# A routed expert layer: zero rows during the last MLP block, unused slots between used ones, and the halves of neighbouring slots interleaved

## The reference

```python
def phi(x):                                   # linear attention, 4 x 8 heads, 576 x 64
    proj = np.einsum('bhsd,df->bhsf', x, w_phi)
    proj = proj - np.max(np.abs(proj), axis=-1, keepdims=True)
    return np.concatenate([np.exp(proj), np.exp(-proj)], axis=-1)
q_p, k_p = phi(q), phi(k)
kv = np.einsum('bhsf,bhsd->bhfd', k_p, v); z = np.sum(k_p, axis=2)
x = (q_p @ kv) / (q_p @ z + 1e-6)             # -> 2304 tokens x 512
h = x @ w_in                                  # dense MLP, 512 -> 2048 -> 512
y = (h * np.clip(h + 3.0, 0.0, 6.0) / 6.0) @ w_out
e_idx = np.argmax(y @ w_gate, axis=1)         # 8 experts, top 1
for e in range(8):                            # 512 -> 1024 -> 512
    m = e_idx == e
    out[m] = gate[m, None] * eom[m, e, None] * (np.maximum(y[m] @ w1[e], 0) @ w2[e])
```

## Time and profile before

| | us |
|---|---|
| runs | 967.49, 962.7, 963.38; median 963.38 |
| profiled execution | 964.04 |
| its span (first to last instruction) | 962.5 |
| PE busy | 869.5 (90%) |
| DVE busy | 580.6 (60%) |
| ACT busy | 388.8 (40%) |
| POOL busy | 74.9 (8%) |

### The profile page before, as it was taken

How to read it: one execution, slowest core, us unless ns; L and a number is a source line. 1 busy time by engine, 2 the same in 40 slices (tenths; PEclk the granted TensorE clock), 3 DMA queues, 4 the chain that set the end, 5 groups by cost and what they waited for, 6 DMA issues and landing times.

```text
span 962.5 us, 20311 instructions
## 1 busy us (share of the span) xinstructions
PE 869.5 (90%) x7480; PEld 574.2 (60%) x7481; DVE 580.6 (60%) x1202; ACT 388.8 (40%) x666; POOL 74.9 (8%) x120
## 2 busy tenths in 40 slices
PE   5999999998899999997999999992499999999990
PEld 3777777777455555553555555552377777777770
DVE  3778788875795987985987987545131322222223
ACT  2445456656456565664656665522010100011011
POOL 1000000000000001001001001011011111111111
PEclk9999999999999999998999999995599999999995
DMA  6243344331565366465266452554317342664110
GB/s 191 92 161 113 132 160 161 128 123 36 192 235 202 143 234 223 162 230 216 97 226 224 156 206 121 201 182 150 103 46 299 137 162 98 228 251 176 44 34 13
DMA packets 44062, 151.36 MB, mean 157 GB/s; under 512 B 7710, under 2 KB 12062, under 8 KB 37856
## 3 DMA queue, kind: packets, MB, share of 16 engines
q1 hardware_dynamic: 38320, 134.14, 39.2%
q0 software_dynamic: 5520, 16.31, 4.9%
q10 hardware_dynamic: 160, 0.07, 0.0%
HBM read 104.72 MB, written 47.21 MB: 158 GB/s over the span
## 4 chain that ended last, share of the span: by engine, by line
PE 57%; PEld 14%; DVE 10%; issue 8%; DMA 4%; PEldq 3%; ACT 2%; SPq 1%; DVEq 0%; POOL 0%; POOLq 0%; ACTq 0%
PE ps L743 19%; PE ps L732 17%; PEld ps L834 10%; PE ps L607 4%; PE ps L634 4%; PE ps L673 3%; PEld ps L846 3%; DVE arena L1087 3%; PE ps L834 2%; PE ps L648 2%; DVE arena L1094 2%; PE ps L846 2%; DMA arena<-split 1%; DVE u_mx L1253 1%; PE ps L661 1%
## 5 line engine op out<-in xcount | busy, mean ns | idle before, releaser
L732 PE MATMUL ps<-arena,w_in_sb 128*128 128x384 f16 x1152 | 203.5, 329 | 6.0 <-issue 6.0
L743 PE MATMUL ps<-w_out_sb,arena 128*128 128x512 f16 x576 | 172.3, 381 | 9.1 <-DVE stage L1341 9.1
L732 PEld LDWEIGHTS ps<-arena,w_in_sb 128*128 128x128 f16 x1152 | 111.4, 99 | 81.7 <-issue 9.2
L1067 ACT ACTIVATE w_in_sb<-ps 128x512 f16<-128x512 f32 x50 | 29.5, 597 | 257.0 <-PE ps L834 241.3
L834 PEld LDWEIGHTS ps<-w_in_sb,arena 128*128 128x128 f16 x2112 | 124.0, 100 | 9.8 <-issue 5.0
L834 PE MATMUL ps<-w_in_sb,arena 128*128 128x128 f16 x2112 | 125.9, 223 | 4.3 <-DMA arena<-split 2.4
L846 PE MATMUL ps<-arena,w_in_sb 128*128 128x512 f16 x528 | 117.5, 379 | 0.0
L743 PE MATMUL ps<-w_out_sb,stage 128*128 128x512 f16 x288 | 109.7, 381 | 0.0
L1442 DVE SCALAR_TENSOR_TENSOR w_in_sb<-ps,w_in_sb 128x512 f16<-128x512 f32 x50 | 34.3, 691 | 113.7 <-ACT w_in_sb L1067 113.7
L743 PEld LDWEIGHTS ps<-w_out_sb,arena 128*128 128x128 f16 x576 | 55.9, 98 | 68.9 <-issue 11.7
L1033 ACT ACTIVATE arena<-relu 128x384 f16<-128x384 f32 x96 | 50.2, 523 | 106.6 <-DVE relu L1336 106.6
(11 more groups left out here) (175 smaller groups left out, 927.5 us busy)
## 6 DMA issues: line engine op xcount, KB each, us to landing
arena<-in_moe_w SPq DMA_DIRECT2D x16, 2048.0 KB, 13.1
split<-arena SPq DMA_DIRECT2D x16, 2048.0 KB, 7.4
arena<-split SPq DMA_DIRECT2D x32, 1024.0 KB, 5.8
arena<-in_qkt SPq DMA_DIRECT2D x15, 576.0 KB, 6.2
stage<-in_moe_w_in SPq DMA_DIRECT2D x16, 512.0 KB, 4.3
stage<-in_moe_w_out SPq DMA_DIRECT2D x16, 512.0 KB, 5.4
w_in_sb<-rows POOLq DMA_DIRECT2D x25, 257.0 KB, 3.0
arena<-in_v SPq DMA_DIRECT2D x32, 128.0 KB, 4.5
```

The costliest lines, as they stand in the source:

```text
L732: last = nc.tensor.matmul(ps[:, HB[f % GB], 0:BN], w_in_sb[:, lw, c, f * P:(f + 1) * P], xt[:, a, c, lx, :], start=c == 0 and lw + lx == 0 ...
L743: last = nc.tensor.matmul(ps[:, YB + r, :], g_sb[lg_][:, f % GB, r * P:(r + 1) * P], w_out_sb[:, lw, f, :], start=f == 0 and lg_ + lw == 0 ...
```

## The change

1. The zero rows of an expert are written as soon as the positions of the last block but one are known: `padrow` is taken in the last MLP block, SP writes 512 rows (`BN + P`) behind each expert's row count so far, and POOL makes the last scatter only when they have landed. `REGION` grows by `BN`. POOL makes `zrow` before its last but one scatter.
2. The tables put the unused slots at positions 2, 4, 6 and so on, as many as there are; `slot_at` is the number of a position among the used ones. The tables that are read later (`slot_inv`) are made behind the release.
3. PE's slot is cut in `hidden_step` and `output_step`. The order is hidden(s + 1), transposes(s + 2), output(s). The output step reads the three table values again. DVE's and POOL's orders follow.
4. w1 of an expert is loaded when the last hidden step of expert e - 2 is done, w2 as before by `eo_done`.

```diff
-REGION = N + P
+REGION = N + BN + P
...
                 load_expert(1, 0, half)
+            sp.wait_ge(zrow_ready, 1)
+            sp.wait_ge(pad_ready, 1)
+            for e in range(E):
+                row = sp.value_load(padrow[0:1, e:e + 1], min_val=0, max_val=DUMMY - BN - P)
+                sp.dma_start(rows[bass.ds(row, BN + P), :].rearrange("(p r) w -> p r w", p=P),
+                             zrow[:, None, :].to_broadcast([P, BT + 1, XW // 2])).then_inc(zeroed, 16)
             sp.wait_ge(y_step, BLOCKS * FC)
             for half in range(2):
                 load_expert(1, 1, half)
 
-            sp.wait_ge(dummy_stored, 16)
-            sp.wait_ge(pad_ready, 1)
-            for e in range(E):
-                row = sp.value_load(padrow[0:1, e:e + 1], min_val=0, max_val=DUMMY - P)
-                sp.dma_start(rows[bass.ds(row, P), :], zrow[:]).then_inc(zeroed, 16)
             sp.wait_ge(table_ready, 1)
             for e in range(2, E):
                 free = sp.value_load(free_at[0:1, e:e + 1], min_val=1, max_val=SLOTS + 1)
+                free1 = sp.value_load(free_w1[0:1, e:e + 1], min_val=1, max_val=2 * SLOTS + 1)
+                sp.wait_ge(eh_done, free1)
+                for half in range(2):
+                    load_expert(e, 0, half)
                 sp.wait_ge(eo_done, free)
                 for half in range(2):
-                    for m in range(2):
-                        load_expert(e, m, half)
+                    load_expert(e, 1, half)
...
-            step(nc.gpsimd.iota(iota_s[:], [[1, SLOTS], [0, E]], base=0, channel_multiplier=0, allow_small_or_imprecise_dtypes=True))
+            step(nc.gpsimd.iota(iota_s[:], [[1, SLOTS]], base=0, channel_multiplier=0, allow_small_or_imprecise_dtypes=True))
+            step(nc.gpsimd.iota(half_s[:], [[1, (SLOTS + 1) // 2], [0, 2]], base=0, channel_multiplier=0, allow_small_or_imprecise_dtypes=True))
+            step(nc.gpsimd.memset(gap_s[:], float(SLOTS + 1)))
+            step(nc.gpsimd.iota(gap_s[:, 2:SLOTS:2], [[1, SLOTS // 2]], base=1, channel_multiplier=0, allow_small_or_imprecise_dtypes=True))
...
-            scatter(BLOCKS - 2)
             pool.wait_ge(x_transposed, BLOCKS * DC)
             step(nc.gpsimd.memset(zrow[:, 0:DM + 1], 0.0))
-            step(nc.gpsimd.iota(zrow[:, DM + 1:DM + 2].bitcast(I32), [[0, 1]], base=NOWHERE, channel_multiplier=1))
-
+            nc.gpsimd.iota(zrow[:, DM + 1:DM + 2].bitcast(I32), [[0, 1]], base=NOWHERE, channel_multiplier=1).then_inc(zrow_ready, 1)
+            pool.wait_ge(zrow_ready, 1)
             pool.dma_start(rows[DUMMY:DUMMY + P, :], zrow[:]).then_inc(dummy_stored, 16)
+            scatter(BLOCKS - 2)
+            pool.wait_ge(zeroed, 16 * E)
             scatter(BLOCKS - 1)
             pool.wait_ge(table_ready, 1)
-            pool.wait_ge(zeroed, 16 * E)
             pool.wait_ge(dummy_stored, 16)
             pool.wait_ge(scattered, 16 * TILES)
...
+            next_load(0, 0)
             with pool.Fori(0, (SLOTS - 3) // 2) as i:
                 for a in range(2):
-                    next_load(i * 2 + a, a)
+                    next_load(i * 2 + (a + 1), 1 - a)
                     store(i * 2 + a, a)
-            next_load(SLOTS - 3, 0)
...
+            pe.drain().then_inc(eh_done, 1)
...
-            def slot(s, a, turn, more=True):
+            def hidden_step(s, a, turn, more=True):
...
                 if more:
                     slot_transposes(s + 1, 1 - a, turn + a)
+
+            def output_step(s, a):
+                parity = pe.value_load(slot_par[0:1, bass.ds(s, 1)], min_val=0, max_val=1)
+                used = pe.value_load(slot_used[0:1, bass.ds(s, 1)], min_val=0, max_val=1)
+                need = pe.value_load(slot_need[0:1, bass.ds(s, 1)], min_val=32, max_val=32 * E)
                 pe.wait_ge(ew2_loaded, need)
                 if not isinstance(s, int) or s > 1:
                     pe.wait_ge(og_ready, s - 1)
...
-            slot(0, 0, 1)
-            slot(1, 1, 1)
-            with pe.Fori(0, (SLOTS - 3) // 2) as i:
-                slot(i * 2 + 2, 0, i + 2)
-                slot(i * 2 + 3, 1, i + 2)
-            slot(SLOTS - 1, 0, SLOTS // 2 + 1, False)
+            hidden_step(0, 0, 1)
+            hidden_step(1, 1, 1)
+            output_step(0, 0)
+            hidden_step(2, 0, 2)
+            output_step(1, 1)
+            with pe.Fori(1, (SLOTS - 3) // 2) as i:
+                hidden_step(i * 2 + 1, 1, i + 1)
+                output_step(i * 2, 0)
+                hidden_step(i * 2 + 2, 0, i + 2)
+                output_step(i * 2 + 1, 1)
+            hidden_step(SLOTS - 2, 1, SLOTS // 2)
+            output_step(SLOTS - 3, 0)
+            hidden_step(SLOTS - 1, 0, SLOTS // 2 + 1, False)
+            output_step(SLOTS - 2, 1)
+            output_step(SLOTS - 1, 0)
 
 
         @block.scalar
...
                 for j in range(2):
-                    act.wait_ge(eh_done, s * 2 + (j + 1))
+                    act.wait_ge(eh_done, s * 2 + (j + 2))
...
+                            nc.vector.tensor_copy(padrow[:], base[:, 0, :]).then_inc(pad_ready, 1)
                     if f not in (0, FC - 1):
                         gate_lo(n, f)
...
+            link(nc.vector.tensor_scalar(unused[:], cnt[:, src, E - 1:E], -1.0, float(SLOTS), ALU.mult, ALU.add))
+            nc.vector.tensor_scalar(slot_gap[:], gap_s[:], unused[:, 0:1], float(2 * SLOTS), ALU.is_le, ALU.mult)
+            link(nc.vector.scalar_tensor_tensor(out=slot_at[:], in0=half_s[:, 0:SLOTS], scalar=unused[:, 0:1], in1=iota_s[:],
+                                                op0=ALU.min, op1=ALU.subtract))
+            link(nc.vector.tensor_tensor(slot_at[:], slot_gap[:], slot_at[:], ALU.subtract))
+
+            link(nc.vector.tensor_tensor(sl[:, 0], slot_at[:, :, None].to_broadcast([P, SLOTS, E]), upto, ALU.is_ge))
             link(nc.vector.tensor_tensor(sl[:, 1], sl[:, 0], upto, ALU.mult))
...
+            link(nc.vector.tensor_scalar(unused_before[:, 2:E], cnt[:, src, 0:E - 2], -2.0, 0.0, ALU.add, ALU.max))
...
+            link(nc.vector.scalar_tensor_tensor(out=unused_before[:, 2:E], in0=unused_before[:, 2:E], scalar=unused[:, 0:1],
+                                                in1=cnt[:, src, 0:E - 2], op0=ALU.min, op1=ALU.add))
+            nc.vector.tensor_scalar(slot_need[:], slot_count[:], 32.0, 32.0, ALU.mult, ALU.add)
+            nc.vector.tensor_scalar(free_w1[:, 2:E], unused_before[:, 2:E], 2.0, 1.0, ALU.mult, ALU.add)
+            link(nc.vector.tensor_scalar(free_at[:, 2:E], unused_before[:, 2:E], 1.0, None, ALU.add))
+            nc.vector.tensor_tensor(e_inv[:], u_pow[:].rearrange("p (e m) -> p e m", m=2)[:, :, 0],
+                                    u_pow[:].rearrange("p (e m) -> p e m", m=2)[:, :, 1], ALU.mult).then_inc(table_ready, 1)
...
             slot_in(0, 0)
-            slot(0, 0, None)
-            slot(1, 1, None)
-            with dve.Fori(0, (SLOTS - 3) // 2) as i:
-                slot(i * 2 + 2, 0, i + 1)
-                slot(i * 2 + 3, 1, i + 1)
-            slot(SLOTS - 1, 0, SLOTS // 2, False)
+            slot_lo(0, 0)
+            slot_in(1, 1)
+            slot_lo(1, 1)
+            slot_in(2, 0)
+            slot_out(0, 0, None)
+            slot_lo(2, 0)
+            slot_in(3, 1)
+            slot_out(1, 1, None)
+            with dve.Fori(1, (SLOTS - 3) // 2) as i:
+                slot_lo(i * 2 + 1, 1)
+                slot_in(i * 2 + 2, 0)
+                slot_out(i * 2, 0, i)
+                slot_lo(i * 2 + 2, 0)
+                slot_in(i * 2 + 3, 1)
+                slot_out(i * 2 + 1, 1, i)
...
```

More of the change, by code:

```diff
@@ L145, in moe_program @@
         slot_par, slot_used, slot_need, parity_i, slot_row, slot_token = (table(SLOTS).bitcast(I32) for _ in range(6))
+        slot_at, slot_gap, slot_count = (table(SLOTS) for _ in range(3))
         og_token = table(2).bitcast(I32)
@@ L175, in moe_program @@
         free_at = sb("free_at", [P, E], I32)
+        free_w1 = sb("free_w1", [P, E], I32)
+        unused = sb("unused", [P, 1])
+        unused_before = sb("unused_before", [P, E])
         expert8 = sb("expert8", [P, E])
@@ L187, in moe_program @@
         cnti = sb("cnti", [P, E], I32)
-        iota_s = sb("iota_s", [P, SLOTS, E])
+        iota_s = sb("iota_s", [P, SLOTS])
+        half_s = sb("half_s", [P, SLOTS + 1])
+        gap_s = sb("gap_s", [P, SLOTS])
         carrier = sb("carrier", [1, 2])
@@ L265, in moe_program @@
         scattered = sem("scattered")
+        zrow_ready = sem("zrow_ready")
         zeroed = sem("zeroed")
@@ L1410, in _ @@
-            link(nc.vector.scalar_tensor_tensor(out=slr[:, 2, :], in0=slr[:, 0, :], scalar=float(REGION), in1=slr[:, 1, :], op0=ALU.mult, op1=ALU.add))
-            link(nc.vector.tensor_scalar(slot_used[:], slr[:, 0, :], float(E), None, ALU.is_lt))
-            link(nc.vector.tensor_scalar(slr[:, 0, :], slr[:, 0, :], float(E - 1), None, ALU.min))
```

(42 more changed lines are left out.)

23 lines of the change are left out of this document (7 added, 16 removed).

## The result

The changed kernel takes 1020.17 us, median of 4 runs (1018.18 to 1020.67), against 963.04 for the kernel before beside it (4 runs, 960.31 to 967.49): ratio 1.0585, 95% interval 1.0542 to 1.0628. The forecast was 1002 with a range of 978 to 1020: right in sign, 18 us short, and at the very edge of its range (0.2 us above its upper end, where the runs themselves spread over 2.5 us). The profiled execution has a span of 1019.0 us, 56.5 more than before.

The account below looks back on a forecast made before the run. PE was taken as busy throughout each used slot (10.99 us) at full clock, with three losses around the slots. The terms summed to +38.9 us on the 962.5 us span, 1001.4, forecast as 1002 us, range 978 to 1020.

Parts of the forecast that it names:

- Term 1: Before 18 outputs that directly follow hidden and transposes: three uncovered value loads idle PE 1.7 us each, +30.6 us.
- R2: Rival: loads ahead of the output are covered, wholly (970 us) or half (986 us); chance 0.12 for both.
- Term 2: Before the hidden step of slot 1, now directly after its transposes: its three loads cost +1.7 us once.
- Terms 3 and 4: Unused positions 2, 4, 6: uncovered loads and drains, +20.8 us; slower clock after four long idle stretches there, +7.8 us.
- Term 5: Late weights of expert 2: w1 is asked for earlier, so the whole loss goes, -4.0 us.
- Term 6: End of the kernel: with a used output last, 24.5 us after its evacuation become 9.8, -14.7 us.
- Term 7: Transition from MLP to slots: earlier but four times larger zero DMAs bring the first row load 3.3 us sooner.
- R4: Rival: zero rows bound the transition at 250 GB/s, +6 instead of -3.3, 1011 us; chance inside the forecast's 0.65.
- R1: Rival: the clock also falls in the regular gaps before outputs, 1017 us, or 1032 if all; chance 0.15.
- R3: Rival: faster, with output loads covered and unused positions skipped cheaply while other work is queued, 945 us; chance 0.05.

Follow-up runs that it names:

- run 1: The kernel before, with PE reading the three table values a second time between transposes and output matmuls: 993.01 us, ratio 1.0355.
- run 2: The changed kernel with the three values packed in one word and both steps' words read ahead of the hidden matmuls: 977.32 us, ratio 1.0183 to the kernel before.
- run 7: As run 2, with one-column matmuls in place of `drain` as an unused slot's signal: 978.56 us, ratio 1.0144 to the kernel before.
- run 8: Run 7 with 128 zero rows late, issued from two queues, and unused slots at 8, 10 and 12: 964.48 us, ratio 1.0009 to the kernel before.
- run 12: Run 8 with an unused slot's hidden step no longer waiting for DVE's copy of its rows: 958.72 us, ratio 0.9950 to the kernel before.
- run 3: The changed kernel with the unused slots put last again: 1013.85 us, ratio 1.0563 to the kernel before.
- run 5: The kernel before with only the changed order of weight loads, w1 first: 958.49 us, ratio 0.9950.
- run 4: The kernel before with the early zero rows alone, 512 per expert: 969.79 us, ratio 1.0116.
- run 6: The changed kernel with the early zero rows undone, 128 per expert written when the last positions are known: 1016.06 us, ratio 1.0546 to the kernel before.
- run 9: The kernel before with w1 first and the eight zero DMAs issued from two queues, SP and ACT: 956.14 us, ratio 0.9921.
- run 11: Run 8 with the unused slots last instead of at 8, 10 and 12: 964.99 us, ratio 1.0024 to the kernel before.

## Why the prediction was right, and where it was short

The step that makes the change slow was forecast as it came: three loads without cover ahead of each regular O. The misses of the other terms nearly all point the same way, so no error hides another; they add up to the 18 us that put the result at the edge of the range.

**Term 1, loads ahead of O (+1.7 a slot).** Right in mechanism and size: +1.79 in the change, +1.70 with the loads alone (run 1), nothing with the loads moved (run 2). This is the larger half of the loss. Every regular gap, 1.41 to 1.86 us, lies in the bracket of 1.2 to 2.1; none has half the price, so R2 falls, whole and half. The Trainium skill (TensorE: Matmul & The Clock Gate, the table of specifications) gives TensorE's queue a depth of 64; no cover beyond the 17 pairs read from the earlier trace rows shows in these gaps.

**Term 2, H(1).** 2.29 for 1.7, and another mechanism: not its loads but DVE's copy of slot 1, which I had put "beside it". The three loads are done at 704.1, the copy ends at 704.88, and the branch is taken at 705.0 (the same in run 2). That the size was near is luck.

**Terms 3 and 4, unused positions and clock.** Forecast 20.8 and 7.8, together 28.6; measured 23.8 of idle (3.24 + 8.17 + 1.74 + 4.38 + 1.90 + 4.38) and 9.3 of slower matmuls, 33.1. Position by position the double one at 765 (6.3 and 2.3 behind it) and the single one at 785 (4.38 and 1.6) came as worked out. The larger part of the miss is the first double one (8.17 + 1.74 for 7.0): a branch past the hidden code that takes 3824 ns the first time and 208 the second. I had such a wait in the upper end alone and not in the value. The rest is position 2 (3.24 and 2.65 behind it, for 2.5 and 1.6). Runs 7 and 8 agree: the same branch takes 4.30 us at the first skip inside the loop in run 7 and 0.22 in run 8, where the loop had been run before, and the stretch shrinks to 1.91. The Trainium skill (Advanced Engine Details and Errata, ISA Cache) gives cache lines of 256 instructions; the skipped step is 2 x 192, so by that figure (an estimate) its end lies outside of the line. No run varies the length that is skipped. What I had given to `drain` in this term belongs in part to DVE's copy (runs 7, 12), and run 3 shows that part of the loss comes with the loop's first pass, unused slots or not.

**Term 5, late weights (-4.0).** Confirmed: H(7), the first of expert 2, starts at 774.91 with no idle time and at full clock, and run 5 has -4.3 (3 to 7) for it alone.

**Term 6, the end (-14.7).** Confirmed: 9.9 to 10.0 from the last evacuation. That the unused slots cost as much in their new place (run 3) is terms 3, 4 and 6 together, and why part 2 of the change gains nothing.

**Term 7, the zero rows (-3.3).** This step failed: +5.5 instead, 8.8 us, half of the whole miss. I divided the bytes by 332 GB/s, the rate of a short window in which few rows were written, and had 28.9 us from the first issue to the last landing (25.4 and what I added to it); it took 35.0, 240 GB/s, with the DMA engines full. The scatter behind it took 7.3 for the 3.2 that I had borrowed from a zero DMA; a piece of w2 was asked for at 678.8 and moved beside it, but no run has this scatter without such a load, so that the load is what slowed it is argued and not shown. The case was R4, priced at +6, which I named but gave too little room. Run 4 has it alone (+0.0116), run 6 takes it away (5.9 us by the trace). The MLP also ended 1.7 us earlier in this execution than in the one before (650.2 for 651.9); by the way from its end to H(0) the step cost 7.2, so that +5.5 flatters it.

**R1, the clock in the regular slots.** It did not come: every H and O from 799.59 on takes 5.52 and 5.34 us, the granted clock is 1.00 (812 to 826), with 1.41 to 1.86 us of idle time ahead of every regular O. It was not far off, though: in run 3 two gaps of 2.44 and 2.62 us in front of used outputs were followed by 8.05 and 7.03 (granted clock 0.66 and 0.76). R3 fell with R2.

The miss adds up: start 8.8, unused positions and clock 4.5, H(1) 0.6, regular slots 1.5; the rest of 17.6 (1019.0 - 1001.4), 2.2, I put down to the transposes of unused slots and the end, without a run that shows it.

## What to carry to other kernels

In these runs a register load cost nothing where the engine's queue held long instructions, and its full time behind short ones; price it by what stands in the queue at that point, and read values that two steps need once, packed, at the covered one. A step moved between the halves of two items loses its cover wherever an item is skipped, and then waits for the copy that was hidden. A transfer made earlier by making it four times larger is priced at the rate of a full stretch, with the transfers behind it; and halving the issue of DMAs brings little when their data takes as long (0.65 of 4.85 us, run 9).

## What was not expected of the hardware

- A branch over code that hadn't been run took 3.82 us (4.30 in run 7, 5.35 in run 2); the same jump took 0.21 the second time, and 0.22 at its first skip in run 8, where the loop had been run. Where it isn't taken over the code, the branch costs 0.07 to 0.09.
- With the DMA engines 0.99 busy, rows of 2056 bytes were written at 240 GB/s beside a scatter and a weight load (284 in all), against 332 in a window with share 0.93.
- The length of one idle stretch did not settle the clock behind it: after 2.29 to 2.31 us the hidden step H(1) took 5.53 in the change and in run 8, and 7.16 in runs 6 and 11 (granted clock 1.00 in the first two, 0.76 and 0.75 in the others); after two idles of 1.91 the output took 5.34 once and 7.03 once (run 8).
